# Solving of a group's systems begins six tiles ahead of its use, first Gram stores on two queues, dense products only ahead of the first tile

## The reference

```python
k_n = k / (np.linalg.norm(k, axis=-1, keepdims=True) + 1e-06)
state = np.zeros((B, H, D, D))              # B 4, H 8, D 48, S 768
for t in range(S):
    kt, vt, bt = (k_n[:, :, t], v[:, :, t], beta[:, :, t, None])
    y[:, :, t] = np.einsum('bhd,bhde->bhe', q[:, :, t], state)
    v_old = np.einsum('bhde,bhd->bhe', state, kt)
    state = state + bt[:, :, :, None] * np.einsum('bhd,bhe->bhde', kt, vt - v_old)
```

## Time and profile before

| what | value |
|---|---|
| median of 3 runs | 1151.85 us (1149.66 to 1152.74) |
| the profiled execution | 1158.75 us, span 1157.0 us |
| PE busy | 999.6 us, 86% of the span |
| DVE busy | 393.2 us, 34% |
| ACT busy | 229.5 us, 20% |
| POOL busy | 143.3 us, 12% |
| mean granted TensorE clock | 0.843 of 2.4 GHz |
| attention | from the start to about 382 us |

### The profile page before, as it was taken

The page is one execution under the profiler, slowest core; times in us unless marked ns, Lnnn a source line. Parts: engine busy times, 40 slices in busy tenths (PEclk is TensorE's granted clock), DMA queues, the critical chain, the costliest instruction groups (busy, mean ns, idle before and its releaser), DMA issues.

```text
span 1157.0 us, 28510 instructions
## 1 busy us (share of the span) xinstructions
PE 999.6 (86%) x11520; PEld 830.4 (72%) x11521; DVE 393.2 (34%) x1391; ACT 229.5 (20%) x625; POOL 143.3 (12%) x214
## 2 busy tenths in 40 slices
PE   4598989998989299999999995338899999999995
PEld 4388888887989178788787874225677777777883
DVE  2756363636321501010111100454453544536000
ACT  2133333323233021212121121000011111111111
POOL 2101010100000011222212221010101111011110
PEclk7759595959576589999999997555899999999998
DMA  7766565644251241111111111030331313314310
GB/s 189 175 149 145 144 151 143 152 124 126 83 153 38 73 130 35 35 35 54 62 35 35 35 35 28 2 131 8 131 123 36 123 49 132 123 29 144 133 39 14
DMA packets 96613, 103.53 MB, mean 89 GB/s; under 512 B 62185, under 2 KB 78711, under 8 KB 96512
## 3 DMA queue, kind: packets, MB, share of 16 engines
q1 hardware_dynamic: 80048, 56.31, 17.3%
q10 hardware_dynamic: 10000, 25.96, 8.4%
q0 software_dynamic: 6464, 19.78, 5.5%
HBM read 81.37 MB, written 21.05 MB: 89 GB/s over the span
## 4 chain that ended last, share of the span: by engine, by line
PE 69%; DVE 11%; DMA 8%; DVEq 4%; issue 3%; SPq 3%; POOL 1%; ACT 0%; POOLq 0%; ACTq 0%
PE M_ps L1176 31%; PE Y_ps L1176 26%; PE T_ps L1241 3%; PE T_ps L1176 3%; DVE outer L637 2%; DMA arena<-inverses 2%; PE Y_ps L1252 2%; DVE lane_inv L642 2%; DVEq L958 2%; SPq L357 2%; DMA inverses<-lane_inv 2%; PE Y_ps L1222 2%; PE T_ps L1348 1%; POOL lane_inv L484 1%; DMA rows_in<-x_rows,gather_now 1%
## 5 line engine op out<-in xcount | busy, mean ns | idle before, releaser
L1176 PE MATMUL M_ps<-xT,arena 128*128 128x128 f32 x2352 | 297.9, 284 | 1.3 <-SPq L415 0.7
L1176 PEld LDWEIGHTS M_ps<-xT,arena 128*128 128x128 f32 x2352 | 283.7, 197 | 14.4 <-SPq L415 1.3
L1176 PE MATMUL Y_ps<-arena,hiddenT 128*128 (+1 forms) x784 | 285.6, 500 | 0.0
L1176 PEld LDWEIGHTS Y_ps<-arena,hiddenT 128*128 128x128 f32 x784 | 139.8, 191 | 70.1 <-issue 0.6
L1123 ACT ACTIVATE hiddenT<-M_ps 128x512 f32<-128x512 f32 x98 | 58.5, 597 | 299.5 <-PE M_ps L1176 299.5
L1176 PEld LDWEIGHTS Y_ps<-chosen_b,reached 128*15 128x15 bf16 x1848 | 50.1, 88 | 47.4 <-DVE reached L726 42.6
L637 DVE SCALAR_TENSOR_TENSOR outer<-lane_inv,lane_scale,lane_gram 128x31 f32<-128x31 f32 (+15 forms) x186 | 74.7, 402 | 21.0 <-POOL lane_scale L479 6.7
L1176 PE MATMUL Y_ps<-chosen_b,reached 128*15 128x8 bf16 x1848 | 57.9, 166 | 25.5 <-DVE reached L726 25.5
L642 DVE TENSOR_TENSOR lane_inv<-lane_inv,outer 128x31 f32<-128x31 f32 (+15 forms) x186 | 63.8, 343 | 14.6 <-issue 0.9
L1176 PE MATMUL M_ps<-k_pad 96*64 96x64 f32 x768 | 40.9, 280 | 30.3 <-DMA k_pad<-k_pad_d 17.5
L1176 PE MATMUL M_ps<-R,arena 64*64 64x48 f32 x768 | 41.5, 262 | 23.7 <-DMA arena<-inverses 23.7
(11 more groups left out here) (201 smaller groups left out, 1039.4 us busy)
## 6 DMA issues: line engine op xcount, KB each, us to landing
arena<-w_d SPq DMA_DIRECT2D x20, 1536.0 KB, 7.4
q_pad<-q_pad_d ACTq DMA_DIRECT2D x22, 384.0 KB, 3.7
k_two<-k_two_d ACTq DMA_DIRECT2D x21, 384.0 KB, 4.2
k_pad<-k_pad_d SPq DMA_DIRECT2D x12, 384.0 KB, 7.4
k_pad<-k_pad_d ACTq DMA_DIRECT2D x12, 384.0 KB, 5.2
x_rows<-x_row SPq DMA_DIRECT2D x24, 192.0 KB, 2.6
v_raw<-v_d ACTq DMA_DIRECT2D x22, 192.0 KB, 2.9
gram<-gram_row SPq DMA_DIRECT2D x96, 32.0 KB, 1.7
```

Of the source, the lines that this page charges most:

```text
L1176: return nc.tensor.matmul(out, lhsT, rhs, start=start, stop=stop)
```

## The change

Five things are edited.

1. **Quarters one tile earlier.** `part(c)` now does the quarter that it did at c + 1. Quarters 0 and 1 of group 1 stand ahead of the loop, quarter 2 behind tile 0. In the loop `scale_lanes` moves ahead of the quarter, `root_lanes` to the end of the tile before.
2. **Turning in two parts.** `store_inverses` at c = 2 modulo 4, `load_inverses` at c = 3 modulo 4.
3. **Gram products' copies** move within a tile from ACT's start to behind the state copies, for tile c + 11 in place of c + 10; their stores on SP stand behind the store of x.
4. **First Gram stores.** The stores of tiles 0 to 3 are shared by SP and ACT, two pieces each; those of tiles 4 to 10 are all on ACT. The first group's inverses are scaled by DVE, not POOL.
5. **Dense products.** The six series of 32 at c = 1 modulo 4 are gone. Ahead of the first `new_values` stand 28, then a wait for the stored inverses, then 12.

```diff
@@ SP, in the loop over tiles
-                if c % GS == GS - 1 and c + 1 < TILES:
-                    turn_inverses((c + 1) // GS)
-                if c + AHEAD - 1 < TILES:
-                    store_gram(c + AHEAD - 1)
-                if (c + AHEAD) % GS == 0 and c + AHEAD <= TILES:
-                    load_lanes((c + AHEAD) // GS - 1)
+                if c % GS == GS - 2 and c // GS + 1 < GROUPS:
+                    store_inverses(c // GS + 1)
+                if c % GS == GS - 1 and c // GS + 1 < GROUPS:
+                    load_inverses(c // GS + 1)
                 if c > 0:
                     store_x(c - 1)
+                if c + AHEAD < TILES:
+                    store_gram(sp, c + AHEAD, range(NB))
+                    if (c + AHEAD) % GS == GS - 1:
+                        load_lanes((c + AHEAD) // GS)
@@ DVE
-                g, quarter = (c + GS + 1) // GS, (c + 1) % GS
+                g, quarter = (c + GS + 2) // GS, (c + 2) % GS
...
             eliminate(0, CH - 6, CH - 1).then_inc(grown, 1)
+            dve.drain()
+            scale_inverses(nc.vector, 0)
             scale_lanes(1)
...
-            for piece in range(len(SLOTS)):
-                part(-1, piece)
+            for c in (-2, -1):
+                for piece in range(len(SLOTS)):
+                    part(c, piece)
@@ ACT, ahead of the loop
             for c in range(GS):
                 copy_gram(c)
+                store_gram(act, c, range(NB // 2, NB))
             root_lanes(0)
-            for c in range(GS, AHEAD - 1):
+            for c in range(GS, AHEAD):
                 copy_gram(c)
+                store_gram(act, c, range(NB))
@@ PE
-                    keep_busy(X_ps[:], 34)
+                    keep_busy(X_ps[:], 28)
+                    pe.wait_ge(inv_out[0], 16)
+                    keep_busy(X_ps[:], 12)
...
-                if c % GS == 1:
-                    keep_busy(KU_ps[0][:, 2 * HALF:512], 32)
```

More of the change, by code:

```diff
@@ L324, in load_values, with store_gram, scale_inverses @@
             engine.dma_start(v_raw[:, c % 2, :, :].rearrange("p h d -> p (h d)"), v_d[c]).then_inc(v_in[c % 2], 16)
+        def store_gram(engine, c, sequences):
+            engine.wait_ge(gram_ready, c + 1)
+            for b in sequences:
+                lanes, own = slice(b * CH, (b + 1) * CH), slice(b % 2 * CH, (b % 2 + 1) * CH)
+                engine.dma_start(gram_d[c].rearrange("h p s -> p h s")[lanes], gram[lanes, c % 3, :, own]).then_inc(
+                    gram_out[c % 3], 16)
+        def scale_inverses(engine, g):
+            inv = lane_inv[:, g % 2, :, :]
+            engine.tensor_tensor(inv, inv, lane_scale[:, g % 2, :].unsqueeze(1).to_broadcast([P, CH, CH]),
+                                 ALU.mult).then_inc(inv_ready, 1)
         def bank(c):
@@ L331, in _ @@
         def _(sp):
[L332 to L337, removed]
             def load_lanes(g):
@@ L346, in load_lanes, with store_inverses @@
                              gram_d[GS * g:GS * g + GS].rearrange("c h (b t) s -> (c h b) (t s)", b=NB)).then_inc(lanes_in[g % 2], 16)
-            def turn_inverses(g):
+            def store_inverses(g):
                 sp.wait_ge(inv_ready, g + 1)
@@ L352, in turn_inverses, with load_inverses @@
                              lane_inv[:, g % 2, :, :].rearrange("p a b -> p (a b)")).then_inc(inv_out[g % 2], 16)
+            def load_inverses(g):
                 sp.wait_ge(inv_out[g % 2], 16 * (g // 2) + 16)
@@ L372, in _ @@
             for c in range(GS):
-                store_gram(c)
+                store_gram(sp, c, range(NB // 2))
             load_lanes(0)
@@ L380, in _ @@
                 load_keys(sp, n)
-            for c in range(GS, AHEAD - 1):
-                store_gram(c)
-                if c % GS == GS - 1:
-                    load_lanes(c // GS)
+            load_lanes(1)
             sp.wait_ge(TT_cleared, 1)
-            turn_inverses(0)
+            store_inverses(0)
+            load_inverses(0)
             for c in range(TILES):
-                if c % GS == GS - 1 and c + 1 < TILES:
-                    turn_inverses((c + 1) // GS)
-                if c + AHEAD - 1 < TILES:
-                    store_gram(c + AHEAD - 1)
-                if (c + AHEAD) % GS == 0 and c + AHEAD <= TILES:
-                    load_lanes((c + AHEAD) // GS - 1)
+                if c % GS == GS - 2 and c // GS + 1 < GROUPS:
+                    store_inverses(c // GS + 1)
+                if c % GS == GS - 1 and c // GS + 1 < GROUPS:
+                    load_inverses(c // GS + 1)
                 if c > 0:
                     store_x(c - 1)
+                if c + AHEAD < TILES:
+                    store_gram(sp, c + AHEAD, range(NB))
+                    if (c + AHEAD) % GS == GS - 1:
+                        load_lanes((c + AHEAD) // GS)
             store_x(TILES - 1)
@@ L479, in square_scales @@
                 nc.gpsimd.tensor_tensor(scale, scale, lane_part[:], ALU.mult).then_inc(lane_scale_ready, 1)
[L481 to L485, removed]
             start_inverses(0)
@@ L493, in _ @@
             for g in range(GROUPS):
-                scale_inverses(g)
+                if g > 0:
+                    pool.wait_ge(grown, g + 1)
+                    scale_inverses(nc.gpsimd, g)
                 if g + 1 < GROUPS:
@@ L716, in _ @@
                     take_out(c, 1)
+                if c % GS == 2 and (c + 6) // GS < GROUPS:
+                    scale_lanes((c + 6) // GS)
                 part(c, 0)
@@ L720, in _ @@
                     token_logits(c - 1)
-                if c % GS == 2 and (c + 6) // GS < GROUPS:
-                    scale_lanes((c + 6) // GS)
             token_logits(TILES - 1)
@@ L1079, in _ @@
             for c in range(TILES):
-                if c + AHEAD - 1 < TILES:
-                    copy_gram(c + AHEAD - 1)
                 if c > 0:
@@ L1091, in _ @@
                     load_channels(act, c + RING)
-                if c % GS == 2 and (c + 6) // GS < GROUPS:
-                    root_lanes((c + 6) // GS)
                 if c + 1 < TILES:
@@ L1098, in _ @@
                                        S_ps[p][0:D2, 0:HD].rearrange("p (h d) -> p h d", d=D)).then_inc(state_ready, 1)
+                if c + AHEAD < TILES:
+                    copy_gram(c + AHEAD)
                 if c + 2 < TILES - 1:
@@ L1109, in _ @@
                     load_values(act, c + 3)
+                if c % GS == 1 and (c + 7) // GS < GROUPS:
+                    root_lanes((c + 7) // GS)
             copy_x(TILES - 1)
@@ L1272, in keep_busy @@
                 for _ in range(times):
-                    mm(out, steady[:, 0:P], steady[:, 0:out.shape[1]])
+                    mm(out, steady[:, 0:P], steady[:])
             for c in range(AHEAD):
```

## The result

The changed kernel takes **1209.87 us** (median of 4 runs, 1207.22 to 1212.22), the kernel before beside it 1150.95: a ratio of 1.051, 95% interval 1.0483 to 1.0537. The forecast was 1195, its range ended at 1206. The direction and the mechanism came out as forecast; the size lies outside the range.

A forecast was written before the change was run, and what follows sets the result against it. PE bounds the kernel, its clock dropping after waits for the turned inverses; without dense products tiles 1 to 23 run low. +40.0 and 3.5 us on 1158.75 give 1202.3, less 6.9 gives 1195; own range 1187 to 1206, widened to 1100 to 1206.

The forecast's parts named there:

- DVE's 22 steps: DVE's list holds 22 steps of group 1 ahead of tile 1's `R`, not 15: 13.3 us plus 7.2 us.
- The first rival: Attention tiles: ordinary products bring the clock back by themselves; 1042 to 1190 us, chance 0.16.
- the 6.9 us taken off at the end: The median stands 6.9 us below the profiled execution of 1158.75, so 1202.3 was lowered to 1195.
- The sum: Whole kernel against the profiled execution: +40.0 us up to `new_values(23, 0)`, about 3.5 behind it, total +43.5, giving 1202.3.
- Term (a): Start, Gram stores of tiles 0 to 3 on two queues: a gain of 2.0 us, bounds 0 and 3.9.
- E: The end of group 0's solving on DVE, 50.75 us before the change, forecast at 48.75.
- Term (b): Start, first inverses scaled on DVE, not POOL: 1.3 us from the end of solving, in place of 2.4.
- Term (c): Start, storing and loading unchanged at 7.0 us: first `new_values` at E + 1.3 + 7.0 = 57.0 us, 3.1 earlier.
- the spell of close to 7 us: PE idles close to 7 us ahead of `new_values(1, 0)`, waiting for `R`; 1.2 GHz follows at once.
- Tile 1's `R`: On DVE, begins at E + 23.5 and serves PE at E + 23.9 = 72.7 us, later than PE asks.
- The tail: From `new_values(23, 0)` to the last logits: 6.5 us now, some 5 of them work; the low level adds about 3.5.
- The second rival: The level survives tile 1, or DVE isn't late there: all tiles high, 1036 to 1042 us, chance 0.04.

The follow-up runs named there:

- experiment 2: The changed kernel with 20 dense products ahead of tile 1's `new_values`, where PE waits for `R`: 1057.10, 1153.58, 1157.71 and 1179.97 us.
- experiment 5: The changed kernel with 20 more dense products ahead of tile 0's `new_values` (60 in place of 40): 1063.11, 1168.22, 1188.17 and 1207.37 us.
- experiment 1: The changed kernel with the six series of 32 dense products put back: 1087.33 us, ratio 0.9436 to the kernel before.
- experiment 3: Two runs: the kernel before without its six series, 1182.97 us, ratio 1.0304; and the kernel before unchanged, profiled again, 1147.86 us.
- experiment 8: Both kernels unchanged, profiled on one chip: the kernel before 1161.78 us, the changed kernel 1203.03 us, ratio 1.0462.
- experiment 7: The changed kernel with 20 dense products ahead of tile 1's `new_values` and no loads of `q_pad` and `k_two` from tile 2 on: 1128.81 us.

## What of the prediction held, and which step failed

**The mechanism held, step by step.** DVE's 22 steps are late for tile 1, PE idles, the clock falls, and ordinary products do not bring it back. The clock's digits, the lost wait for `arena<-inverses` and the tiles (16.43 and 14.32 us, against 16.6 and 14.3) are as forecast. Experiments 2 and 5 shorten the idle spell, in two ways, and in the profiled run of each the level passes tile 1; experiment 1 gives only the series back, and the ratio to the kernel before goes from 1.051 to 0.944. The loss thus needs both halves: a fall, and nothing dense behind it. The first rival (ordinary products bring the clock back) is refuted for the mix of products in these tiles by 350.15 of 351.80 us busy at 1.2 GHz. The Trainium skill's rule, "TensorE: Matmul & The Clock Gate", section "Why this matters for your kernels", would have had the level return in that stretch; the trace disagrees. What spoke for the rival was the rise at 47.2 us behind Gram products alone. That rise didn't come again: in the three other profiles of this order (experiments 3 and 8) the level rose between 53.0 and 54.7 us, inside the dense products.

**The step that failed: the 6.9 us taken off at the end.** The sum against the profiled execution was 1202.3; I then took off what that execution stood above the median, and got 1195. That offset wasn't a constant overhead. It was the kernel before losing the clock at tile 0: its profile is at 0.50 from 60.90 to 88.00 us, the one of 1147.86 us (experiment 3) is at 1.00 there, and the one of 1161.78 us (experiment 8) falls at tile 0 again. Runs without a profile fit this: beside experiment 8 the five of 1143.31 to 1148.78 us had a mean clock of 0.849 to 0.852, the two of 1154.88 and 1160.00 us one of 0.842. The changed kernel is low from tile 1 on in each of its profiles and has no such good course, so none of the 6.9 us carries over: its profiled run took 1209.91 us, its median is 1209.87. Without that step the forecast would have been 1202.3. Experiment 8 gives 1203.03, 0.7 us from the sum and 8.0 from the forecast. So close a sum is partly luck: tile 1's `new_values` began 2.8 us later than summed (75.52), and the tiles, the tail and the mixtures together gave most of it back.

**The rest of the miss.** 1209.87 - 1202.3 = 7.6 us. In the first profiles the second mixture's longer rounds are about 4 of them, and experiment 8 shows that they don't belong to the change. The other 3 to 4 are the attention's: the last logits begin 427.47 - 380.84 = 46.6 us later than before, where the sum had 43.5. By its terms:

- Term (a), the start: E came at 49.40, not 48.75; the gain is 1.35 us, not 2.0.
- Term (b), the scaling: 1.3 us, as taken.
- Term (c), 57.0 us for the first `new_values`: it was 63.68. I had the 40 dense products end by then, but PE began them only at 53.35 and at 1.2 GHz. This costs nothing by itself, since PE idles at tile 1 anyhow. With `R` 4.6 us later and tile 0 6.7 us later than summed, the spell of close to 7 us becomes 7 + 4.6 - 6.7 = 4.9, and it was 4.72.
- Tile 1's `R`: it begins at 76.83 against E + 23.5 = 72.3. Of these 4.6 us E makes 0.65, and the two waits for ACT make 3.67, which the sum had at nothing: it had even taken the 0.58 us of waiting of before off. The rest is 0.3 us in DVE's own work. I had listed the split stores as a gain on SP and never counted them on ACT's queue, which I moved them to. That is the mis-sized term: +4.6 us, of which the queue on ACT makes 3.67.
- The tiles from 1 to 23: 418.71 - 77.32 = 341.4 us, against 342.4. The tail: 427.47 - 418.71 = 8.8 us, where 5.7 and 3.5 make 9.2. The 3.5 was too much by its own figures: 5 us of work at 1.09 / 0.67 add 3.1.

**The second rival** (the level survives tile 1) came true only in kernels where that wait was filled. Its price of 1036 to 1042 was too low: the best runs of such kernels gave 1057.10 and 1063.11, and in the profiles of these kernels the first `new_values` came at 63.77 and 65.85 us in place of 57.0.

What stays open: what the spells without a visible cause are; why a spell of 1.5 us drops the clock in one run and not in another; how stores on SP with group 1's load in its old place would do; and what makes the mixture's rounds 1 us longer on some occasions.

## What to carry to other kernels

A stretch of dense work with an unread result does two jobs, to bridge a wait and to bring the clock back. Take it out only once no idle spell of any kind is left in front of ordinary work, and look for the new ones: here the reordering ended six waits, and the one new wait at tile 1 then cost more than all six. Work moved ahead of an engine's first deadline must be summed in that engine's queue, the DMA issues of the engine that takes them over included. An offset between a profiled execution and the median may be a difference in course and not overhead: ask which stretch it lies in before carrying it over.

## What the runs showed of the hardware

- PE at 2.4 GHz stood idle for up to 1.53 us at times with nothing to wait for that the profile shows; at a DMA share of 0.55 in place of 0.83 there were none in 75 us, and at 1.2 GHz (share 0.41) one kernel was busy for 350.15 of 351.80 us. In two kernels one came at the same instruction (145.07 and 143.38 us).
- A spell of 1.3 to 1.6 us was followed by 1.2 GHz in experiments 1, 2 and 7, and in experiment 5 it was not. Ahead of tile 0 of the kernel before, 2.70 and 2.80 us were followed by it, 0.90 and 0.19 us were not. The four runs of experiment 5, a kernel without series, took 1063 to 1207 us on one chip.
- Small f32 products kept PE busy for 350.15 of 351.80 us at 1.2 GHz and the level did not rise; behind 32 dense bf16 products it did, at 91.6 us of the kernel before.
- 28 stores of 32 KB took 26.86 us to issue on SP (DMA share 0.80), and four took 8.12 us on ACT at worst (share 1.06). Ahead of that, with a share of 0.46, four had taken 1.93 us on SP.
- The same program's mixture rounds took 47.43 us on one occasion and 48.43 on another.
